# Four of the ten local row minima subtracted by GpSimd with one exponential for them, small copies moved to ScalarE, and the side work of VectorE placed behind the totals

## The chip, the core and the metric

The kernel runs on one NeuronCore of one Trainium2 chip. Five engines work side by side, each through its own instructions in program order: TensorE (PE, with its weight loads as PEld), VectorE (DVE), ScalarE (ACT), GpSimd (POOL), and SyncE (SP), which here only issues DMAs. They wait for each other through semaphores written out by hand. The metric is the time of the whole program in microseconds (us) on the device; lower is better. The kernel before took 819.59 us (median of three runs, 819.48 to 819.81).

## The reference

Three parts follow each other, all in float32. First comes attention over 4 batches x 8 heads, 576 positions, head size 64, in two forms that are added:

```python
q_d, k_d, v_d = (mean over groups of 4 positions of q, k, v)
out_d = sm_attn(q_d, k_d, v_d)              # 144 x 144 scores per head
out_up = np.repeat(out_d, factor, axis=2)
mask = np.abs(pos[:, None] - pos[None, :]) < factor      # a band of 7 keys
scores = np.where(mask, scale * q @ k^T, -1e9)
attn = exp(scores - max); attn /= (sum + 1e-9)
x = out_up + attn @ v
```

Then `h = (x @ w1) * (x @ w2) @ w3 @ w_out` on 2304 tokens of width 512 with inner width 1024, and last `silu(h @ w_in) @ w_out2` with inner width 2048.

## The kernel before, in words

**Layout.** Two heads are one pair, and there are 16 pairs. The attention is a software pipeline of 17 steps: in `step(s)` each engine does its share of pair s and the rest of pair s-1. Behind it run 48 sets of seven products (line 993) and the layers that follow them, which fill TensorE from about 165 us on. The product of `moe_w3` with `moe_w_out` is folded into the attention steps (line 1076), a twelve-matmul portion in each from step 4 on, so that TensorE has work there.

**The local attention of a pair** is computed on ten blocks of 64 queries by 64 keys (five groups of two per head; the tile `prob`, 128 x 640). DVE copies the negated, scaled scores out of PSUM and adds the mask (`mask_local`, line 718), and then takes the minimum of each block's rows (line 723, tile `low`, 128 x 10). ACT turns each of the ten blocks into exponentials with `low` as its bias and lets the accumulator add up the row (line 484, tile `tot`). DVE adds 1e-9 and inverts (`totals_local`, lines 739 and 741), POOL multiplies the whole tile by the inverse (line 402), PE transposes it (line 1128), ACT copies it back (`copy_pt`), and PE multiplies with the values (line 1151).

**The downsampled attention** goes the same way on a smaller scale: `qkd` from DVE (line 707), scores on PE (line 1095), maximum and its scaling on DVE (lines 729 and 733), four exponentials on ACT (line 473), totals on DVE (lines 746 and 749), the normalisation on POOL (line 408), transposes on PE (line 1120), `copy_ptd` on ACT, the product on PE (line 1137), a copy to `od` on DVE (`take_down`, line 753), and the sum of both forms into `x` (`take_local`, line 762).

**The order within one step** is fixed by the code:

- PE: local scores of pair s, downsampled scores of s, local transposes of s-1, nine fold matmuls, downsampled transposes of s-1, three fold matmuls, both products of s-1.
- DVE: x of pair s-2, mask and minimum of s, downsampled totals of s-1 (it makes `invd`), maximum of s, `qkd` of s+1, in some steps the two copies of a fold result (`take_w3o`) and one half of the first product's operands (table `EXTRA`), local totals of s, `od` of s-1.
- ACT: the fold's weights (`w3_high`), `copy_pt`, six local exponentials, `copy_ptd`, four local exponentials, four downsampled ones, in two steps a copy of weights for the first product (table `HIGHS`).
- POOL: sums over the values (lines 380 to 389), in eight steps a weight sum (line 364, table `SUMS`), the local normalisation of s, `w3_low` (line 369), the downsampled normalisation of s (line 408), which waits for `invd` from the next DVE step.

## Time and profile before

| what | us |
|---|---|
| median of the runs | 819.59 |
| the profiled execution | 821.13 |
| its span in the trace | 819.2 |
| PE busy (share) | 794.3 (97%) |
| DVE busy | 600.9 (73%) |
| ACT busy | 354.9 (43%) |
| POOL busy | 279.3 (34%) |

The profiled execution lies 1.54 us above the median of the runs, and 1.93 us of it lie outside the span. The page shows the span in 40 slices of 20.5 us. In the first seven, which hold the attention, DVE, ACT and POOL stand at 5 to 9 tenths and the DMA share at 3 to 8; after them PE stands at 9 and the rest falls off. TensorE's granted clock is at 9 tenths or more in every slice but the second (7 tenths).

```text
PE   7699899999999999999999999999999999999998
DVE  5898997687676776876669677679767769756644
ACT  6878877333352232443246323334422344432331
POOL 6778877432313333133213123113113212311100
PEclk9799999999999999999999999999999999999999
```

### The profile page before, as it was taken

The page shows a single profiled execution, that of the slowest core. Times are in us where ns is not written, and L with a number is a line of the kernel's source. Part 1 is how long each engine was busy: PE and PEld are TensorE (multiplying, and loading weights), DVE is VectorE, ACT ScalarE, POOL GpSimd, SP SyncE. Part 2 cuts the span into 40 slices and gives each one's busy share as a digit, 9 for nine tenths or more (in the row PEclk, how much of TensorE's full clock was granted, in tenths as well). Part 3 has the DMA queues.
Part 4 walks back from the last instruction along what each step waited for, and adds up shares of the span by engine and source line. Part 5 has one row for each costly group of instructions (what it writes and reads, how often), then busy time and mean ns, then how long its engine had stood idle before and what let it go on. Part 6 is the DMA issues. An engine that isn't in the chain of part 4 may idle for free.

```text
span 819.2 us, 13951 instructions
## 1 busy us (share of the span) xinstructions
PE 794.3 (97%) x5393; PEld 714.9 (87%) x5393; DVE 600.9 (73%) x957; ACT 354.9 (43%) x863; POOL 279.3 (34%) x342
## 2 busy tenths in 40 slices
PE   7699899999999999999999999999999999999998
PEld 6577777899999899999999889888888988988887
DVE  5898997687676776876669677679767769756644
ACT  6878877333352232443246323334422344432331
POOL 6778877432313333133213123113113212311100
PEclk9799999999999999999999999999999999999999
DMA  8475753011111111101103122122312112412102
GB/s 302 150 243 171 237 159 120 29 52 33 46 52 52 30 49 52 45 33 52 51 27 130 51 81 74 52 78 78 129 56 99 52 51 78 154 52 78 51 1 78
DMA packets 23041, 69.84 MB, mean 85 GB/s; under 512 B 2496, under 2 KB 2496, under 8 KB 22976
## 3 DMA queue, kind: packets, MB, share of 16 engines
q1 hardware_dynamic: 22832, 68.36, 25.7%
q8 instruction: 43, 0.70, 0.4%
q10 hardware_dynamic: 144, 0.59, 0.2%
q14 instruction: 22, 0.18, 0.1%
HBM read 64.23 MB, written 4.72 MB: 84 GB/s over the span
## 4 chain that ended last, share of the span: by engine, by line
PE 84%; POOL 5%; DVE 4%; DMA 2%; issue 2%; ACT 2%; SPq 0%; POOLq 0%
PE ps L993 42%; PE ps L1051 24%; PE ps L1022 12%; PE ps L1076 2%; DMA wn<-in_w 2%; POOL prob L402 2%; POOL w3t L369 1%; POOL prob_d L408 1%; PE ps L1120 1%; DVE wa L681 1%; PE ps L1151 1%; ACT prob L484 1%; POOL vd L385 1%; DMA qk<-in_qk 1%; PE ps L1137 1%
## 5 line engine op out<-in xcount | busy, mean ns | idle before, releaser
L993 PE MATMUL ps<-xb,wa 128*128 128x384 f32 x2016 | 406.9, 339 | 1.9 <-DVE a L821 1.4
L993 PEld LDWEIGHTS ps<-xb,wa 128*128 128x128 f32 x2016 | 356.6, 189 | 24.3 <-DVE a L821 2.1
L364 POOL TENSOR_TENSOR rw<-rw 128x256 f32<-128x256 f32 x192 | 167.9, 893 | 450.0 <-DMA rw<-in_sets 339.8
L821 DVE TENSOR_TENSOR mu<-ps,mu 128x384 f32<-128x384 f32 x132 | 73.2, 555 | 121.7 <-PE ps L993 121.2
L1022 PE MATMUL ps<-g,r 128*128 128x512 f32 (+1 forms) x576 | 124.9, 338 | 1.6 <-issue 1.6
L575 ACT ACTIVATE a<-a 128x384 f32<-128x384 f32 x72 | 37.9, 526 | 189.1 <-DVE a L821 189.1
L1051 PE MATMUL ps<-w2h_even,g 128*128 128x512 f32 x432 | 113.2, 394 | 0.0
L1051 PE MATMUL ps<-w2h_odd,g 128*128 128x512 f32 x432 | 112.5, 393 | 0.0
L681 DVE TENSOR_TENSOR wa<-rw,wa 128x1024 fp32r<-128x1024 f32 x96 | 107.0, 1114 | 3.0 <-ACT wa L427 2.7
L1022 PEld LDWEIGHTS ps<-g,r 128*128 128x128 f32 x576 | 97.7, 188 | 10.1 <-issue 2.2
L1051 PEld LDWEIGHTS ps<-w2h_odd,g 128*128 128x128 f32 x432 | 79.9, 188 | 11.9
L1051 PEld LDWEIGHTS ps<-w2h_even,g 128*128 128x128 f32 x432 | 79.9, 188 | 11.7
L821 DVE TENSOR_TENSOR a<-ps,mu 128x384 f32<-128x384 f32 x108 | 59.9, 555 | 37.2 <-PE ps L993 36.2
L427 ACT ACTIVATE wa<-rw 128x1792 fp32r<-128x1792 f32 (+2 forms) x49 | 81.5, 1663 | 0.0
L427 ACT ACTIVATE mu<-ps 128x384 f32<-128x384 f32 x48 | 23.3, 486 | 111.0 <-PE ps L993 111.0
L848 DVE TENSOR_TENSOR g<-a,g 128x384 fp32r<-128x384 f32 x96 | 64.1, 668 | 3.3
L427 ACT ACTIVATE g<-a 128x384 fp32r<-128x384 f32 x48 | 25.3, 526 | 80.2 <-DVE a L827 63.4
L484 ACT ACTIVATE prob<-prob,low 128x64 f32<-128x64 f32 x160 | 53.3, 338 | 6.9 <-DVE low L723 6.6
L1076 PE MATMUL ps<-r,w3t 128*128 128x512 f32 x192 | 51.0, 404 | 0.0
L846 DVE CAST g<-a 128x384 fp32r<-128x384 f32 x96 | 45.3, 472 | 0.0
L1076 PEld LDWEIGHTS ps<-r,w3t 128*128 128x128 f32 x192 | 34.0, 189 | 5.8
L833 DVE TENSOR_TENSOR g<-a,g 128x384 fp32r<-128x384 f32 x48 | 32.9, 690 | 0.4
(75 smaller groups left out, 744.2 us busy)
## 6 DMA issues: line engine op xcount, KB each, us to landing
rw<-in_sets SPq DMA_DIRECT2D x48, 512.0 KB, 3.6
w2r<-in_w_out SPq DMA_DIRECT2D x24, 512.0 KB, 3.5
qk<-in_qk SPq DMA_DIRECT2D x15, 576.0 KB, 5.5
vg<-in_vg SPq DMA_DIRECT2D x16, 336.0 KB, 6.0
vw<-in_vw SPq DMA_DIRECT2D x16, 320.0 KB, 3.0
out<-osb SPq DMA_DIRECT2D x18, 256.0 KB, 2.3
wn<-in_w SPq DMA_DIRECT2D x16, 256.0 KB, 5.1
raw<-in_w_out SPq DMA_DIRECT2D x2, 1024.0 KB, 9.5
```

Of the source, the lines that this page charges most:

```text
L364: nc.gpsimd.tensor_tensor(blocks[:, o, :], blocks[:, a, :], blocks[:, b, :], op).then_inc(done, 1)
L427: return nc.scalar.activation(o, a, ACT.Copy)
L484: e = nc.scalar.activation(pr, pr, ACT.Exp, bias=low[:, u, n:n + 1], scale=-1.0, accum_out=tot[:, u, n:n + 1])
L575: nc.scalar.activation(q, q, ACT.Silu).then_inc(g_act, 1)
L681: e = nc.vector.tensor_tensor(wa[:, k % 2, 1, blocks, :], rw[:, k % 2, 1 + blocks.start:1 + blocks.stop, :], wa[:, k % 2, 0, blocks, :].bi ...
L821: nc.vector.tensor_tensor(o, half_bank(k, i), term, ALU.add).then_inc(sum_ready, 1)
L846: nc.vector.tensor_copy(g[:, 0, j % 2, q // 2, to], a4[:, q, :]).then_inc(g_hi, 1)
L848: nc.vector.tensor_tensor(g[:, 1, j % 2, q // 2, to], a4[:, q, :], g[:, 0, j % 2, q // 2, to].bitcast(F32), ALU.subtract).then_inc(g_lo, 1)
L993: e = nc.tensor.matmul(ps[:, (k + i) % 2, 0:TH], wa[:, k % 2, l, A_SLOT[i], a * P:(a + 1) * P], xb[:, i, r, a, :], start=(i in (0, 1, 4) a ...
L1022: e = nc.tensor.matmul(o, r2[:, m + MT // 2 * f, l, b * P:(b + 1) * P], g[:, r, n % 2, f, to], start=(first and p == 0 and not (rest and b ...
L1051: e = nc.tensor.matmul(ps[:, 2 + tb, :], g[:, l, j % 2, q // 2, at], w2h[j % 2][:, q // 2, r, :], start=(c == 0 and a < 2 and p == 0), sto ...
L1076: e = nc.tensor.matmul(ps[:, fold_bank(q), :], w3t[:, l, a, :], r3[:, a, r, :], start=(a == 0 and p == 0), stop=(a == MT - 1 and p == 2))
```

## The change

Nothing changes on PE; the work moves among DVE, ACT and POOL inside the attention steps.

- **Local exponentials.** ACT now does only the first six blocks (groups 0 to 2) with bias and accumulator. For the last four (128 x 256) POOL subtracts `low` (`shift_local`), ACT takes one exponential over all of them, and DVE sums their rows (a TENSOR_REDUCE into `tot`). In POOL's order the subtraction for pair s+1 stands between `w3_low` and the downsampled normalisation of pair s.
- **Small copies.** The scaling of the downsampled maximum, the copy to `od` and the first copy of each fold result go from DVE to ACT, behind the late exponential.
- **Side work behind the totals.** On DVE the rest of `take_w3o` and the `EXTRA` halves come after `totals_local` instead of before it. The weight loads, weight sums and copies for the first product come one step earlier (`SUMS`, `HIGHS`), and `EXTRA` has a new order.

The core of the diff:

```diff
-        SUMS = (6, 10)
-        HIGHS = (8, 10)
-        EXTRA = {9: ("tokens", 0), 10: ("tokens", 1), 11: ("weights", 0), 12: ("tokens", 2), 13: ("weights", 1),
+        SUMS = (5, 9)
+        HIGHS = (7, 9)
+        EXTRA = {8: ("weights", 0), 10: ("tokens", 0), 11: ("weights", 1), 12: ("tokens", 1), 13: ("tokens", 2),
                  14: ("tokens", 3)}
...
+            def shift_local(s):
+                u = s % 2
+                pool.wait_ge(low_l, s + 1)
+                late = prob[:, u, LATE:NG, :, :].rearrange("p g h k -> p (g h) k")
+                nc.gpsimd.tensor_tensor(late, late, low[:, u, 2 * LATE:10, None].broadcast_to([P, 10 - 2 * LATE, BW]),
+                                        ALU.subtract).then_inc(shifted, 1)
...
+                if s == 0:
+                    shift_local(0)
+                    shift_local(1)
...
                 for q in splits_of(s + 1)[:1]:
                     w3_low(q)
+                if s > 0 and s + 1 < PAIRS:
+                    shift_local(s + 1)
                 pool.wait_ge(inv_d, s + 1)
...
                 def exps_down():
+                    act.wait_ge(maxd, s + 1)
+                    nc.scalar.activation(lowd16[:, u, :], lowd[:, u, :], ACT.Copy, scale=-D ** -0.5 / POOL ** 2
+                                         ).then_inc(low_d, 1)
                     act.wait_ge(low_d, s + 1)
...
+                def exps_late():
+                    act.wait_ge(shifted, s + 1)
+                    late = prob[:, u, LATE:NG, :, :].rearrange("p g h k -> p (g h k)")
+                    nc.scalar.activation(late, late, ACT.Exp, scale=-1.0).then_inc(exp_s, 1)
+
+                def take_down():
+                    act.wait_ge(summed_d, s)
+                    after(act, x_ready, 2 * (s - 2))
+                    copy_act(od[:, (s - 1) % 2, :], ps[:, pO, 0:SD]).then_inc(od_ready, 1)
...
+                if s > 2:
+                    exps_local()
+                if s > 0:
+                    copy_ptd()
+                if s == 2:
+                    exps_local()
+                if s != 1:
+                    exps_late()
+                for q in halves_of(s):
+                    if q % 2 == 1:
+                        take_w3o(q // 2)
...
                 exps_down()
+                if s > 0:
+                    take_down()
...
             def totals_local(s):
                 u = s % 2
+                dve.wait_ge(exp_s, s + 1)
+                nc.vector.tensor_reduce(tot[:, u, 2 * LATE:10].rearrange("p (g h) -> p g h", h=2),
+                                        prob[:, u, LATE:NG, :, :], AX.X, ALU.add).then_inc(sum_l, 1)
                 dve.wait_ge(exp_l, s + 1)
+                dve.wait_ge(sum_l, s + 1)
...
+                totals_local(s)
+                if s == 0:
+                    totals_down(0)
                 for q in halves_of(s):
                     if q % 2 == 1:
                         take_w3o(q // 2)
...
-                totals_local(s)
-                if s == 0:
-                    totals_down(0)
-                else:
-                    take_down(s - 1)
```

On POOL, in the steps with a weight sum, these rows stood before (`w3t` is `w3_low`, the second `prob` row's place is the local normalisation, `prob_d` the downsampled one, `vt` the next pair's values):

```order
L364 TENSOR_TENSOR rw<-rw 128x256
L402 TENSOR_TENSOR prob<-prob,inv 128x640
L369 TENSOR_TENSOR w3t<-wn,w3t 128x512
L408 TENSOR_TENSOR prob_d<-prob_d,invd 72x4x144
L380 TENSOR_TENSOR vt<-vg 112x384
```

And these stand there now:

```order
L367 TENSOR_TENSOR rw<-rw 128x256
L415 TENSOR_TENSOR prob<-prob,inv 128x640
L372 TENSOR_TENSOR w3t<-wn,w3t 128x512
L380 TENSOR_TENSOR prob<-prob,low 128x256
L423 TENSOR_TENSOR prob_d<-prob_d,invd 72x4x144
L390 TENSOR_TENSOR vt<-vg 112x384
```

One row is new, the subtraction, directly ahead of the downsampled normalisation. On ACT, a step with a fold result read before (`pt` and `ptd` are the copies of the transposes, the last row opens the next step):

```order
L427 ACTIVATE pt<-ps 128x384
L427 ACTIVATE pt<-ps 128x256
L484 ACTIVATE prob,tot<-prob,low 128x64 x6
L427 ACTIVATE ptd<-ps 112x2x3x72
L484 ACTIVATE prob,tot<-prob,low 128x64 x4
L473 ACTIVATE prob_d,totd<-ps,lowd 72x144 x4
L427 ACTIVATE w3t<-wn 128x512
```

The same step now, here one that also holds the weight copy of `HIGHS` (step 7):

```order
L442 ACTIVATE pt<-ps 128x384
L442 ACTIVATE pt<-ps 128x256
L506 ACTIVATE prob,tot<-prob,low 128x64 x6
L442 ACTIVATE ptd<-ps 112x2x3x72
L513 ACTIVATE prob<-prob 128x256
L442 ACTIVATE r<-ps 128x512
L490 ACTIVATE lowd<-lowd 72x4
L495 ACTIVATE prob_d,totd<-ps,lowd 72x144 x4
L442 ACTIVATE od<-ps 128x144
L442 ACTIVATE wa<-rw 128x1024
L442 ACTIVATE w3t<-wn 128x512
```

Four blocks became one row, and three small rows came in around the downsampled exponentials. On DVE, a step with a fold result and an `EXTRA` half, from `qkd` to the next `x`, read before (step 11):

```order
L707 TENSOR_REDUCE qkd<-qk 128x288
L698 CAST r<-ps 128x512
L700 TENSOR_TENSOR r<-ps,r 128x512
L681 TENSOR_TENSOR wa<-rw,wa 128x1024
L739 TENSOR_SCALAR tot<-tot 128x10
L741 RECIPROCAL inv<-tot 128x10
L753 COPY od<-ps 128x144
L762 TENSOR_TENSOR x<-ps,od 128x288 x2
```

And now:

```order
L743 TENSOR_REDUCE qkd<-qk 128x288
L772 TENSOR_REDUCE tot<-prob 128x4
L776 TENSOR_SCALAR tot<-tot 128x10
L778 RECIPROCAL inv<-tot 128x10
L736 TENSOR_TENSOR r<-ps,r 128x512
L719 TENSOR_TENSOR wa<-rw,wa 128x768
L795 TENSOR_TENSOR x<-ps,od 128x288 x2
```

The totals moved ahead of the side work, which now stands directly in front of the next step's `x`; two copies left.

## Rows read from the trace of the kernel before

**Rows 1.** Windows: us, busy us per engine (instructions), PEclk, DMA share, GB/s.

```profile
45.00:60.00 15.00, 14.11 (x230) 11.64 (x228) 14.18 (x29) 12.34 (x60) 12.19 (x17) 1.00 0.66 213
180.00:195.00 15.00, 15.00 (x86) 14.23 (x85) 9.37 (x15) 3.13 (x4) 3.36 (x5) 1.00 0.23 71
```

**Rows 2.** Waits, 45 to 135 us: us in total, times, longest.

```profile
PEld ps L1120 <- POOL prob_d L408: 6.0, 11, 1.1
```

**Rows 3.** Timeline, step 6: start us, us, engine, line, operation, out<-in.

```profile
56.13 0.27 PE L1108 MATMUL ps<-qk 64*64 64x64 f32 x1
56.53 0.82 DVE L762 TENSOR_TENSOR x<-ps,od 128x288 f32<-128x288 f32 x2 [0.36 <-PE ps L1151]
58.18 0.82 DVE L723 TENSOR_REDUCE low<-prob 128x10 f32<-128x640 f32 x1
58.21 1.30 POOL L369 TENSOR_TENSOR w3t<-wn,w3t 128x512 fp32r<-128x512 f32 x1 [0.80 <-ACT w3t L427]
58.92 0.62 DVE L746 TENSOR_SCALAR totd<-totd 72x4 f32<-72x4 f32 x1
59.82 1.14 POOL L408 TENSOR_TENSOR prob_d<-prob_d,invd 72x576 f32<-72x576 f32 x1 [0.31 <-DVE invd L749]
62.07 0.34 ACT L484 ACTIVATE prob<-prob,low 128x64 f32<-128x64 f32 x1
63.40 0.36 ACT L473 ACTIVATE prob_d<-ps,lowd 72x144 f32<-72x144 f32 x1
63.53 0.58 DVE L739 TENSOR_SCALAR tot<-tot 128x10 f32<-128x10 f32 x1 [1.28 <-ACT prob L484]
64.26 0.27 PE L1108 MATMUL ps<-qk 64*64 64x64 f32 x1
64.82 0.63 ACT L427 ACTIVATE w3t<-wn 128x512 fp32r<-128x512 f32 x1
```

**Rows 4.** Timeline, starts in steps 5, 7, 8 and 15.

```profile
47.78 0.27 PE L1108 MATMUL ps<-qk 64*64 64x64 f32 x1
48.88 1.26 POOL L402 TENSOR_TENSOR prob<-prob,inv 128x640 f32<-128x640 f32 x1
...
67.05 0.16 DVE L746 TENSOR_SCALAR totd<-totd 72x4 f32<-72x4 f32 x1
67.49 1.14 POOL L408 TENSOR_TENSOR prob_d<-prob_d,invd 72x576 f32<-72x576 f32 x1 [0.56 <-DVE invd L749]
71.93 0.27 PE L1108 MATMUL ps<-qk 64*64 64x64 f32 x1
...
129.53 0.27 PE L1108 MATMUL ps<-qk 64*64 64x64 f32 x1
132.76 1.14 POOL L408 TENSOR_TENSOR prob_d<-prob_d,invd 72x576 f32<-72x576 f32 x1 [0.67 <-DVE invd L749]
```

**Rows 5.** Groups by shape, 45 to 135 us: busy us, mean ns, idle before.

```profile
L402 POOL TENSOR_TENSOR prob<-prob,inv 128x640 f32<-128x640 f32 x11 | 13.9, 1259 | 6.2 <-DVE inv L741 6.0
L364 POOL TENSOR_TENSOR rw<-rw 128x256 f32<-128x256 f32 x8 | 5.8, 729 | 0.6
L427 ACT ACTIVATE pt<-ps 128x256 f32<-128x256 f32 x11 | 4.2, 379 | 0.0
```

**Rows 6.** Timeline around 94 us.

```profile
94.11 1.84 POOL L385 TENSOR_TENSOR vd<-vt 96x64 f32<-96x64 f32 x3
94.27 0.94 DVE L675 TENSOR_TENSOR tr<-x,tr 128x768 f32<-128x768 f32 x1
```

**Rows 7.** Timeline, steps 2 and 3.

```profile
29.07 0.82 DVE L762 TENSOR_TENSOR x<-ps,od 128x288 f32<-128x288 f32 x2
29.31 0.38 ACT L473 ACTIVATE prob_d<-ps,lowd 72x144 f32<-72x144 f32 x1
33.16 1.14 POOL L408 TENSOR_TENSOR prob_d<-prob_d,invd 72x576 f32<-72x576 f32 x1
```

**Rows 8.** Windows of the start.

```profile
33.00:45.00 12.00, 10.03 (x121) 8.70 (x121) 9.55 (x16) 8.84 (x43) 9.65 (x12) 0.65 0.34 114
```

More of the change, by code:

```diff
@@ L170, in attention_then_mlps @@
             sem("pooled"), sem("maxd"), sem("low_d"), sem("masked"), sem("low_l"), sem("x_ready"))
+        shifted, exp_s, sum_l = sem("shifted"), sem("exp_s"), sem("sum_l")
         added_d, added_l, inv_d, inv_l = sem("added_d"), sem("added_l"), sem("inv_d"), sem("inv_l")
@@ L180, in attention_then_mlps @@
         s1_ready, s2_ready, s3_ready, s4_ready = sem("s1_ready"), sem("s2_ready"), sem("s3_ready"), sem("s4_ready")
-        wa_hi, wa_lo = sem("wa_hi"), sem("wa_lo")
+        wa_hi, wa_lo, wa_first = sem("wa_hi"), sem("wa_lo"), sem("wa_first")
         prod, m1_ready, sum_ready, c11_taken = sem("prod"), sem("m1_ready"), sem("sum_ready"), sem("c11_taken")
@@ L452, in first_weights_high @@
                     act.wait_ge(s1_ready, 1)
-                    copy_act(wa[:, 0, 0, 0:4, :], rw[:, 0, 1:5, :])
+                    copy_act(wa[:, 0, 0, 0:4, :], rw[:, 0, 1:5, :]).then_inc(wa_first, 1)
                 else:
@@ L457, in first_weights_high, with take_w3o @@
                     copy_act(wa[:, 0, 0, 4:7, :], rw[:, 0, 5:8, :]).then_inc(wa_hi, 1)
+            def take_w3o(m):
+                act.wait_ge(w3_mul, 2 * m + 2)
+                copy_act(r2[:, m, 0, :], ps[:, fold_bank(2 * m), :]).then_inc(w3o_hi, 1)
             def w3_high(q):
@@ L477, in exps_down, with exps_local @@
                     e.then_inc(exp_d, 1)
-                def exps_local(groups):
+                def exps_local():
                     act.wait_ge(low_l, s + 1)
-                    for g in groups:
+                    for g in range(LATE):
                         for h in range(2):
@@ L514, in step @@
                     tokens_high(0, 2)
+                    take_w3o(MT - 2)
                     w3_high(HALVES - 1)
+                    take_down()
                     act.wait_ge(w3_lo, HALVES)
@@ L522, in step @@
                     tokens_high(0, 6)
+                    take_w3o(MT - 1)
                     return
@@ L526, in step @@
                     w3_high(q)
+                if s < 2:
+                    exps_local()
+                if s == 1:
+                    exps_late()
+                if s > 0:
+                    copy_pt()
+                if s > 2:
[3 more added lines that the diff above has]
+                if s == 2:
+                    exps_local()
+                if s != 1:
+                    exps_late()
+                for q in halves_of(s):
+                    if q % 2 == 1:
+                        take_w3o(q // 2)
                 if s == 0:
-                    exps_local(range(NG))
                     act.wait_ge(blank, 2)
-                elif s == 1:
-                    exps_local(range(LATE))
-                    copy_pt()
-                    copy_ptd()
-                    exps_local(range(LATE, NG))
-                elif s == 2:
-                    copy_pt()
-                    copy_ptd()
-                    exps_local(range(NG))
-                else:
-                    copy_pt()
-                    exps_local(range(LATE))
-                    copy_ptd()
-                    exps_local(range(LATE, NG))
                 exps_down()
+                if s > 0:
+                    take_down()
                 for n in W_OUT.get(s, ()):
@@ L678, in weights_low @@
                 blocks = (slice(0, 4), slice(4, 7))[half]
-                if half == 0:
+                if half == 0 and k > 0:
                     dve.wait_ge(wa_hi, k + 1)
@@ L731, in max_down @@
                                         AX.X, ALU.max).then_inc(maxd, 1)
-                dve.wait_ge(maxd, s + 1)
-                nc.vector.tensor_scalar(lowd16[:, u, :], lowd[:, u, :],
-                                        -D ** -0.5 / POOL ** 2, None, ALU.mult).then_inc(low_d, 1)
             def totals_local(s):
                 u = s % 2
+                dve.wait_ge(exp_s, s + 1)
+                nc.vector.tensor_reduce(tot[:, u, 2 * LATE:10].rearrange("p (g h) -> p g h", h=2),
+                                        prob[:, u, LATE:NG, :, :], AX.X, ALU.add).then_inc(sum_l, 1)
                 dve.wait_ge(exp_l, s + 1)
+                dve.wait_ge(sum_l, s + 1)
                 nc.vector.tensor_scalar(tot1[:, u, :], tot[:, u, :], 1e-9, None, ALU.add).then_inc(added_l, 1)
@@ L793, in step @@
                     else:
+                        if n == 0:
+                            dve.wait_ge(wa_first, 1)
+                        else:
+                            dve.wait_ge(wa_hi, 1)
                         weights_low(0, n)
-                totals_local(s)
-                if s == 0:
-                    totals_down(0)
-                else:
-                    take_down(s - 1)
             pool_pair(0)
@@ L809, in _ @@
             take_w3o(MT - 2)
-            take_down(PAIRS - 1)
             take_local(PAIRS - 1)
```

8 lines of the change are left out of this document (1 added, 7 removed).

## The prediction

> **What bounds the kernel now.** I read the windows first. From 180 us on TensorE is busy 15.00 of 15.00 us, while in the attention it is busy 14.11 of 15 [rows 1]. The change touches only the attention and its two ends, so what is to win or lose lies there. The waits tell what TensorE lacks: its loads of the downsampled transposes wait for POOL's downsampled normalisation in all of eleven steps [rows 2]. The timeline tells how this sets the pace.
>
> I call S the start of a step's local scores on PE and N the start of the downsampled normalisation (L408) inside that step. In step 6, S is 56.13, N is 59.82 and the next S is 64.26 [rows 3]: N comes 3.69 us after S, and the next S 4.44 us after N. In step 7, S is 64.26, N 67.49 and the next S 71.93 [rows 3, 4]: 3.23 and again 4.44. In each of the ten steps from 5 to 14 it is 4.44 within 0.01, whatever DVE and ACT had beside it. So a step lasts L + 4.44, with L the lag from S to N, and the attention is priced by L alone. Ten steps take 129.53 - 47.78 = 81.75 us [rows 4], so their ten lags sum to 81.75 - 44.4 = 37.35; step 15 adds 132.76 - 129.53 = 3.23. The eleven lags sum to 40.6, 3.69 each, with 3.23 the shortest.
>
> What makes up L is seen in step 6 [rows 3]: `x` of pair s-2 starts 0.40 us after S (the end of the previous products), the row minimum starts at 2.05 and ends at 2.87, then come the downsampled totals on DVE, `invd`, and N. In step 7 the totals take 0.16 us and N is 0.36 after the minimum's end [rows 4]; in step 6 they take 0.62 [rows 3], because `w3_low` runs on POOL until 59.51 and the totals end only at 59.54.
>
> **The late exponentials.** Four blocks take 63.40 - 62.07 = 1.33 us on ACT [rows 3]. One instruction of 256 elements took 0.38 as a copy [rows 5]; I take 0.42 for the exponential. DVE's new sum over 256 elements is 256/640 of the minimum's 0.82, 0.33, to 0.43 with a fixed part; I take 0.43. Local totals come 0.5 us earlier. This is worth nothing by itself: the local normalisation feeds the local transposes and `w3_low`, and neither of them is what PE waits for last. In step 6 everything local is over before the wait at N.
>
> **The subtraction on POOL.** 256 elements cost between 0.50 (256/640 of 1.26) and 0.73 (the 128x256 weight sum) [rows 5]; I take 0.60. It cannot start before the minimum of pair s+1 is done, and it stands in front of N. So a step that is otherwise on time has N at 2.87 + 0.05 + 0.60 + 0.03 = 3.55 after S, where the best one now has 3.23. What hid behind it before, totals and `invd`, took 0.36. Both ends: 3.45 to 3.68. Nothing covers it, since PE already waits at exactly this place.
>
> **The small copies on ACT.** Counted from N: `copy_ptd` is over at 62.07 - 59.82 = 2.25 [rows 3]. Then come the late exponential (0.42), in odd steps the first fold copy (512 elements, 0.60 from the 0.38 of 256 [rows 5]), the scaled maximum with its hand-over (0.30, by the smallest ACT rows 0.2 each), four downsampled exponentials (64.82 - 63.40 = 1.42 [rows 3]), and the copy to `od` (0.28). It ends at N + 4.67 in even steps and N + 5.27 in odd ones. The next `x` starts at N + 4.44 + 0.40 = 4.84 today and needs `od`. So behind even steps nothing is late; behind odd steps it starts at about 5.35, 0.5 late, and with it mask, minimum, subtraction and N. Lags of steps 6, 10, 12, 14 and 8 become 4.05. In steps 8 and 10 the weight copy of `HIGHS` (1024 and 768 elements, by the 0.63 of 512 [rows 3] some 1.06 and 0.85 us) stands between the copy to `od` and `w3_high`, so `w3_low` and with it the subtraction come later still: ACT is through `w3_high` at N + 5.27 + 1.06 + 0.63 = 6.96, `w3_low` ends at 8.3, which is 3.9 after S, and N is at 4.55 (step 8), by the same count 4.35 (step 10). In step 12 DVE itself, behind a fold result and a weight half, is through only about 0.1 after ACT; I leave it at 4.05. Even steps: 3 x 4.05 + 4.55 + 4.35 = 21.05.
>
> **The side work behind the totals.** DVE's row of totals, counted from N: the late exponential is over at 2.67, the sum at 3.15, and `inv` is ready at 3.6, if the small totals instruction is not held up. In step 6 it was: it took 0.58 us instead of 0.16 [rows 3], beside a weight sum on POOL. If it is held until the weight sum ends, `inv` is ready at N + 4.55. Then the `EXTRA` half (0.94 for tokens [rows 6], up to 1.3 for 1024 elements of weights) is behind it and ends at 5.0 to 6.0, past the 4.84 at which the next `x` is due. In the kernel before this time lay where DVE waited for the exponentials anyway, in the even steps. Steps 9, 11 and 13 have such a half in front: unhindered totals give 3.75, 3.55, 3.55, held-up totals 4.65, 4.3, 4.15. A token half beside a POOL instruction also stretched three short additions to 1.84 us [rows 6], which speaks for the later ones. I take values about halfway: 4.1, 3.9, 3.85. Step 5 is bound by POOL: the local normalisation starts 1.10 after S [rows 4], it and `w3_low` (1.26 and 1.30) end 3.6 after S, and the subtraction follows: 4.3. Steps 7 and 15 have 3.55. Odd steps: 4.3 + 3.55 + 4.1 + 3.9 + 3.85 + 3.55 = 23.25.
>
> The Trainium skill, page "SBUF — State Buffer", section "Who interferes with whom", says that VectorE's tensor_scalar in a two-port mode and a GpSimd instruction lock each other out of a shared pair of ports for a whole instruction, and that an addition with both inputs in SBUF contends with GpSimd's reads. The rows of the totals (0.16 alone, 0.58 and 0.62 beside POOL) and the 1.84 us [rows 3, 4, 6] agree. By that rule the subtraction, which follows `w3_low` without a gap, could also keep the downsampled totals out until it has ended, which is the third rival's price.
>
> **The start.** In steps 2 and 3 ACT is the engine that is never idle. The downsampled exponentials of step 2 end about 29.67, the copy to `od` now comes after them, and `x` starts at about 29.85 instead of 29.07 [rows 7]: 0.78 late. The subtraction's excess over the totals' 0.36 adds 0.3 and the one in step 2 shifts the row before by another 0.3. N of step 3, now 33.16 [rows 7], comes 1.1 to 1.4 later; I take 1.4. In the window from 33 to 45 us the granted clock reads 0.65 [rows 8]: some 8.4 of the 12 us at its lower level, 1.2 GHz, beginning while PE waits for this N. I expect the same stretch again.
>
> **The end.** After the last step ACT reaches `w3_high` 0.35 later than now, behind the same fold copy and `od`; the rest of the way to the first products is PE's and DVE's own and unchanged: 0.35.
>
> **The sum.** Steps 5 to 15: 21.05 + 23.25 - 40.6 = +3.7. Start +1.4, end +0.35. Together +5.45 on the profiled 821.13, so 826.6; the profile lies 1.54 above the median, and against 819.59 this is 825.0.
>
> **The rivals.**
>
> *Faster: the gain of even distribution.* The mean lag stands 0.46 over the shortest, since in some steps DVE comes late from side work and in others the totals wait for `w3_low`, as in step 6. If ACT keeps up (its copies cost less than I count) and the totals are never held up, every lag is 3.45: 11 x 3.45 = 37.95, which is 2.65 less than 40.6. If besides PE is kept busy enough at the start for the clock not to fall, the twelve us of [rows 8] lose about 2 us of slow matmuls. That gives 815 to 817. For it: DVE loses the scaling, a copy and half of a fold result, against a sum of 0.43. Against it: in no step does the subtraction vanish, and `x` behind odd steps needs ACT to save 0.5 us. 15 in 100 including its milder forms.
>
> *No change.* The late steps recover (-1.5 to -2.6) and the start pays 1.0 to 1.4: 818.5 to 820. It needs the same on ACT as the first rival. 15 in 100.
>
> *Slower still: the totals are starved.* If the downsampled totals are held out behind `w3_low` and the subtraction in every step where `w3_low` runs until the minimum's end, they and `invd` add 0.3 us after the subtraction in six or seven steps (+2), and the held-up values of steps 9, 11 and 13 add 1.25: 828.3. It decides from the point where `w3_low` ends later than 2.87 after S. 20 in 100.
>
> *That the change doesn't do what it says* would show in POOL's order, and the rows of the order have the subtraction where the code puts it.
>
> **How the numbers follow.** The forecast, 822 to 827 around 825.0, has 50 in 100. Faster than before by over 0.2% (1.6 us, about what can be told from no change here) is 0.15, within it 0.15, slower 0.70. The range goes from 817.5, which takes in no change and the mild half of the first rival, to 829, which takes in the starved case. The forecast's own range is 822 to 827.
>
> **What the changed profile would show.** Right: N minus S at 3.5 or more in every step from 5 to 15, next S still N + 4.44; `x` waiting for ACT's `od` in steps 6, 8, 10, 12 and 14; POOL's subtraction at about 0.6 us directly ahead of N. Wrong: lags under 3.4 (the subtraction is cheaper or hidden), a distance from N to the next S that differs from 4.44 (something else than N sets the pace), or no half clock near 35 us.

## The result and the profile after

The changed kernel takes 822.75 us (median of seven runs, 822.29 to 824.02); the kernel before took 819.81 in the seven runs beside it (819.46 to 822.24). The ratio is 1.0032, with a 95% interval from 1.0020 to 1.0044: slower by 2.6 to 2.9 us. The forecast was 825.0 and "slower"; the direction held, the size is about half of the 5.45 us that was summed up. The profiled execution is itself one of 822.75 us, with a span of 821.0 (before: 819.2).

The page shows that work has moved as the diff says: POOL gained 9.8 us of busy time, DVE lost 9.6 and ACT 5.8.

```profile
span 821.0 us, 13901 instructions
PE 792.2 (97%) x5393; PEld 712.1 (87%) x5393; DVE 591.3 (72%) x933; ACT 349.1 (43%) x791; POOL 289.1 (35%) x358
```

The windows of the changed kernel that answer to [rows 1, 8] (columns as there). From 180 us on nothing changed. In the attention PE is busy 0.43 us less of the 15, and POOL 1.59 more. Half clock at the start came again, shorter (0.72 against 0.65).

```profile
33.00:45.00 12.00, 9.11 (x114) 7.64 (x114) 10.06 (x18) 8.12 (x37) 10.11 (x13) 0.72 0.36 118
45.00:60.00 15.00, 13.68 (x229) 11.21 (x230) 12.00 (x23) 11.14 (x48) 13.78 (x19) 1.00 0.62 199
180.00:195.00 15.00, 15.00 (x86) 14.18 (x85) 9.31 (x14) 3.13 (x4) 2.88 (x4) 1.00 0.24 71
```

The wait of [rows 2], 45 to 135 us, in the changed kernel. TensorE's loads still wait eleven times for POOL's downsampled normalisation, now 9.3 us in place of 6.0:

```profile
PEld ps L1154 <- POOL prob_d L423: 9.3, 11, 1.2
```

Step 6 in the changed kernel's timeline, against [rows 3] (start, us, engine, line, operation):

```profile
57.08 0.27 PE L1142 MATMUL ps<-qk 64*64 64x64 f32 x1
57.37 0.28 ACT L442 ACTIVATE od<-ps 128x144 f32<-128x144 f32 x1
57.68 0.82 DVE L795 TENSOR_TENSOR x<-ps,od 128x288 f32<-128x288 f32 x2 [0.76 <-ACT od L442]
...
60.07 0.16 DVE L783 TENSOR_SCALAR totd<-totd 72x4 f32<-72x4 f32 x1
60.24 0.62 POOL L380 TENSOR_TENSOR prob<-prob,low 128x256 f32<-128x256 f32 x1 [0.71 <-DVE low L759]
60.81 1.15 POOL L423 TENSOR_TENSOR prob_d<-prob_d,invd 72x576 f32<-72x576 f32 x1
...
65.25 0.27 PE L1142 MATMUL ps<-qk 64*64 64x64 f32 x1
...
68.04 0.16 DVE L783 TENSOR_SCALAR totd<-totd 72x4 f32<-72x4 f32 x1
...
68.77 1.15 POOL L423 TENSOR_TENSOR prob_d<-prob_d,invd 72x576 f32<-72x576 f32 x1
```

S is 57.08, `x` waits for ACT's `od` and starts 0.60 after S (before 0.40), the subtraction runs 0.62 directly ahead of N, N is 60.81, and the next S, 65.25, is N + 4.44. Step 7 is the best one: N at 68.77 is 3.52 after S, where it was 3.23 [rows 3, 4]. The totals take 0.16 in both: they get in before the subtraction.

The groups by shape of the changed kernel, 45 to 135 us, beside [rows 5] (busy us, mean ns of one, idle before):

```profile
L415 POOL TENSOR_TENSOR prob<-prob,inv 128x640 f32<-128x640 f32 x11 | 17.6, 1601 | 0.9 <-DVE inv L778 0.9
L380 POOL TENSOR_TENSOR prob<-prob,low 128x256 f32<-128x256 f32 x11 | 6.8, 616 | 3.6 <-DVE low L759 3.2
L772 DVE TENSOR_REDUCE tot<-prob 128x4 f32<-128x256 f32 x11 | 4.6, 419 | 11.4 <-ACT prob L513 11.4
L513 ACT ACTIVATE prob<-prob 128x256 f32<-128x256 f32 x11 | 4.5, 408 | 0.0
L442 ACT ACTIVATE od<-ps 128x144 f32<-128x144 f32 x11 | 3.1, 285 | 0.0
L442 ACT ACTIVATE r<-ps 128x512 fp32r<-128x512 f32 x5 | 3.0, 597 | 0.0
L783 DVE TENSOR_SCALAR totd<-totd 72x4 f32<-72x4 f32 x11 | 2.6, 240 | 0.0
L490 ACT ACTIVATE lowd<-lowd 72x4 f32<-72x4 f32 x11 | 2.1, 193 | 0.0
```

Every new operation has the price that was forecast (0.62 for 0.60, 0.41 for 0.42, 0.42 for 0.43, 0.29 for 0.28, 0.60 for 0.60). What has grown is the local normalisation, 1259 to 1601 ns in the mean.

**The balance by steps.** The lag is S to N, read from the timeline (last digits rounded):

| step | 5 | 6 | 7 | 8 | 9 | 10 | 11 | 12 | 13 | 14 | 15 | sum |
|---|---|---|---|---|---|---|---|---|---|---|---|---|
| before | 3.91 | 3.69 | 3.23 | 3.30 | 3.82 | 4.00 | 3.60 | 4.26 | 3.57 | 4.01 | 3.23 | 40.6 |
| forecast | 4.3 | 4.05 | 3.55 | 4.55 | 4.1 | 4.35 | 3.9 | 4.05 | 3.85 | 4.05 | 3.55 | 44.3 |
| changed | 4.02 | 3.73 | 3.52 | 3.95 | 3.94 | 3.73 | 3.68 | 3.74 | 3.68 | 4.57 | 3.52 | 42.1 |
| `x` after S | .40 | .60 | .40 | .61 | .83 | .60 | .57 | .62 | .57 | 1.45 | .39 | |

From N to the next S it is 4.43 or 4.44 in each step from 5 to 14. Against the span's start, the two timelines differ so: the first S came 0.49 later (6.54 against 6.05; it waits for the DMA of `qk`, which the change does not touch, and lies between 5.86 and 6.61 in the fourteen profiles of this document), the way from there to step 5 grew by 0.36 (42.09 against 41.73), the lags by 1.46, and the way from N of step 15 (135.10 against 132.76) to the last downsampled normalisation by 0.26. That makes 2.6, of which 0.5 is not the change's. Then the trace of before loses some of it by itself: its granted clock falls once more at the first products. The two traces there, before first (windows as above):

```profile
160.00:162.00 2.00, 1.22 (x4) 1.22 (x5) 1.19 (x3) 0.00 (x0) 1.92 (x3) 0.74 0.31 72
162.00:164.00 2.00, 2.00 (x7) 2.00 (x7) 0.56 (x1) 0.00 (x0) 0.53 (x2) 0.50 0.48 190
```

```profile
160.00:162.00 2.00, 1.82 (x9) 1.18 (x8) 2.00 (x4) 0.00 (x0) 1.44 (x2) 1.00 0.00 0
162.00:164.00 2.00, 0.73 (x4) 0.73 (x5) 1.68 (x3) 0.00 (x0) 2.00 (x2) 1.00 0.21 25
```

The first sets' `a` start 2.5 us apart (160.2 and 162.7), those at 166.8 and 167.8 still 1.0. So 1.5 us of the difference is missing there, because the profiled execution of before had this second stretch; none of the thirteen other profiles has one at this place. That execution, 821.13, also lay 1.3 to 1.5 above the medians of its kernel. Of the 2.6 to 2.9 us between the medians the change's own rows explain 2.1 (0.36 + 1.46 + 0.26, without the later first S); the rest, 0.5 to 0.8, has no row. That is the grain of such a balance: from the first matmul of the sets to the last of `w2h_even`, work that no kernel here changes, the profiles take 653.2 to 654.2 us (654.8 in before's), and below, attention and median differ by up to 1.2 us either way.

### The profile page after: what moved, and what is told of

It is laid out like the page before. It is cut to its first block, busy times and chain, and to the rows that moved or that the text cites. A ratio compares the mean times of both kernels' runs of the same rounds, so it can differ in the third digit from the quotient of the medians.

```text
span 821.0 us, 13901 instructions
## 1 busy us (share of the span) xinstructions
PE 792.2 (97%) x5393; PEld 712.1 (87%) x5393; DVE 591.3 (72%) x933; ACT 349.1 (43%) x791; POOL 289.1 (35%) x358
## 4 chain that ended last, share of the span: by engine, by line
PE 83%; DVE 6%; ACT 4%; POOL 3%; issue 2%; DMA 2%; SPq 0%; DVEq 0%; POOLq 0%; ACTq 0%
PE ps L1027 42%; PE ps L1085 24%; PE ps L1056 12%; POOL prob_d L423 2%; PE ps L1110 1%; PE ps L1154 1%; DVE low L759 1%; DVE prob L754 1%; ACT prob_d L495 1%; DMA wn<-in_w 1%; PE ps L1185 1%; DVE x L795 1%; ACT ptd L442 1%; DVE wa L719 1%; DMA qk<-in_qk 1%
## 5 line engine op out<-in xcount | busy, mean ns | idle before, releaser
L506 ACT ACTIVATE prob<-prob,low 128x64 f32<-128x64 f32 x96 | 32.1, 338 | 8.3 <-DVE low L759 8.1
```

## The experiments

The twelve kernels were timed against the kernel before in four sets (e1 to e4, e5 to e8, e9 to e11, e12); the median of before was 820.81, 820.16, 820.23 and 820.32 in them, and 819.81 beside the changed kernel. So medians of different sets are up to 1.0 us apart for nothing, and the ratios are the safer comparison. "Start" is from the first S to S of step 5 (41.73 before, 42.09 changed), "lags" the sum of steps 5 to 15.

| kernel | median | ratio (95%) | start | lags | shortest lag |
|---|---|---|---|---|---|
| changed | 822.75 | 1.0032 (1.0020 to 1.0044) | 42.09 | 42.1 | 3.52 |
| e1 | 821.22 | 1.0003 (0.9994 to 1.0012) | 41.28 | 41.8 | 3.23 |
| e2 | 822.80 | 1.0029 (1.0017 to 1.0040) | 41.87 | 42.7 | 3.52 |
| e3 | 825.61 | 1.0059 (1.0046 to 1.0071) | 43.19 | 43.6 | 3.52 |
| e4 | 830.17 | 1.0116 (1.0103 to 1.0130) | 43.49 | 47.7 | 3.95 |
| e5 | 825.25 | 1.0062 (1.0049 to 1.0075) | 41.82 | 44.6 | 3.52 |
| e6 | 827.45 | 1.0084 (1.0071 to 1.0098) | 41.43 | 46.7 | 3.23 |
| e7 | 820.64 | 1.0006 (0.9997 to 1.0014) | 40.79 | 40.8 | 3.23 |
| e8 | 820.61 | 1.0001 (0.9992 to 1.0010) | 40.76 | 40.6 | 3.23 |
| e9 | 819.33 | 0.9989 (0.9980 to 0.9998) | 41.61 | 39.2 | 3.23 |
| e10 | 818.47 | 0.9977 (0.9968 to 0.9986) | 40.14 | 39.4 | 3.23 |
| e11 | 817.80 | 0.9971 (0.9960 to 0.9983) | 39.90 | 40.3 | 3.23 |
| e12 | 819.67 | 0.9995 (0.9986 to 1.0004) | 39.90 | 41.7 | 3.23 |

**e1_shift_behind: the subtraction behind the downsampled normalisation.** From the changed kernel, on POOL:

```diff
                 for q in splits_of(s + 1)[:1]:
                     w3_low(q)
-                if s > 0 and s + 1 < PAIRS:
-                    shift_local(s + 1)
                 pool.wait_ge(inv_d, s + 1)
...
                                         ).then_inc(norm_d, 1)
+                if s > 0 and s + 1 < PAIRS:
+                    shift_local(s + 1)
```

> The changed kernel with one edit: POOL's subtraction for pair s+1 stands behind the downsampled normalisation of pair s instead of in front of it. In the changed kernel the start of that normalisation (N) comes 3.52 us or more after the start of the local scores (S), where the kernel before had 3.23. Theory 1 (the subtraction in front of N is what lengthens the steps): the shortest lag goes back to 3.23, the eleven lags of steps 5 to 15 lose about 0.25 us each, and with the start the kernel gains about 3 us: 819.5 to 820. Theory 2 (the copies on ACT and the side work on DVE are what counts): the lags stay where they are and the time stays at 822.5. Against theory 1 speaks only that the values and the local normalisation on POOL come 0.6 us later, which nobody waits for last.

It took 821.22, by its ratio level with the kernel before (1.0003), as expected. The shortest lag is back at 3.23, so the subtraction is what lifted it by 0.29 (0.32 was forecast). But the trace shows less than the "0.25 us in each of eleven lags": the start is 0.8 shorter and the lags as a whole fell by 0.3 only, 1.1 us together where the ratios are 2.4 us apart. In steps 5, 9 and 11 to 13 the lags rose. Step 11 of this kernel, with S at 96.74:

```profile
97.77 1.25 POOL L415 TENSOR_TENSOR prob<-prob,inv 128x640 f32<-128x640 f32 x1
98.98 1.27 POOL L372 TENSOR_TENSOR w3t<-wn,w3t 128x512 fp32r<-128x512 f32 x1
99.53 0.75 DVE L783 TENSOR_SCALAR totd<-totd 72x4 f32<-72x4 f32 x1
100.57 1.14 POOL L421 TENSOR_TENSOR prob_d<-prob_d,invd 72x576 f32<-72x576 f32 x1 [0.32 <-DVE invd L786]
```

The local normalisation starts 1.03 after S (the subtraction delays the exponential, that delays `inv`, and a weight sum comes in between), `w3_low` runs until 100.25, and the downsampled totals take 0.75 instead of 0.16. The gain of 0.29 per step turned into a wait for `w3_low`.

**e2_extra_front: the halves ahead of the local totals.** From the changed kernel, on DVE:

```diff
+                if s in EXTRA: ...          # the whole block
                 totals_local(s)
...
-                if s in EXTRA: ...
```

> The changed kernel with the halves for the first product (table EXTRA) ahead of the local totals on DVE again, the fold result's second half still behind them. Theory 2: step 14, whose lag is 4.57 us in the changed kernel with x 1.45 us after S, falls to about 3.6, step 9 from 3.94 to 3.7, and the local normalisation on POOL takes 1.26 us again in steps 8 and 10 to 12 where it now takes 2.0: 1.3 to 2 us gained, 821. Theory 1: these halves were only a small part, 0.5 us or less gained.

It took 822.80, no different from the changed kernel. Step 14 fell from 4.57 to 3.73, and POOL's local normalisation takes 1.26 us again in every step, both as expected. But `inv` came later, and with it POOL's local normalisation and `w3_low`. Step 11 of this kernel, with S at 98.17:

```profile
100.38 1.29 POOL L372 TENSOR_TENSOR w3t<-wn,w3t 128x512 fp32r<-128x512 f32 x1
100.95 0.74 DVE L783 TENSOR_SCALAR totd<-totd 72x4 f32<-72x4 f32 x1
...
102.20 1.15 POOL L423 TENSOR_TENSOR prob_d<-prob_d,invd 72x576 f32<-72x576 f32 x1
```

The totals (0.74) are kept out beside `w3_low`, the subtraction follows them, and the lag is 4.03, not 3.68. Steps 9 and 11 to 13 rose by 0.29 to 0.35 each. So both orders on DVE cost the same, in other steps, and the forecast's term "halves behind totals" bought nothing that could be had back by undoing it.

**e3_od_on_dve: the copy to `od` back on DVE, at the end of its row.**

```diff
-                if s > 0:
-                    take_down()                       # ACT
...
+                if s > 0:
+                    take_down(s - 1)                  # DVE, behind the EXTRA half
```

> The changed kernel with the copy to od back on DVE, at the end of its step. In the changed kernel x starts 0.60 us after S in steps 6, 8, 10 and 12 and 0.40 in steps 7 and 15, where only ACT's od is in the way. If ACT's lateness is the cause (theory 2, copies): these four go to 0.40 and the kernel gains 0.8 to 1 us: 822. If the copies cost what the prediction had (0.5 us in each of five steps): 2.5 us. Theory 1: under 0.5 us, since DVE's own row ends little earlier.

A gain of about 1 us was expected; it took 2.9 us more (2.2 by the ratios). Steps 6 and 10, the ones where only ACT's `od` was late, fell by 0.2 as expected (3.73 to 3.53 and 3.54). In steps 9 and 11 to 14 the copy stands behind the fold result and the half, and `x` starts 0.88 to 1.77 after S. The other part of the loss is at the start, which is 1.10 longer: N to the next S takes 7.89 us in step 3, where it was 6.49. At that place on DVE the copy costs more than ACT's late one; where it costs nothing is seen in e7.

**e4_no_subtraction: ten exponentials on ACT again, all else as changed.** This kernel keeps the small copies and the side order, without `shift_local`, the joint exponential and DVE's sum over it:

```diff
-                if s > 0 and s + 1 < PAIRS:
-                    shift_local(s + 1)
...
                 def exps_late():
-                    act.wait_ge(shifted, s + 1)
-                    late = prob[:, u, LATE:NG, :, :].rearrange("p g h k -> p (g h k)")
-                    nc.scalar.activation(late, late, ACT.Exp, scale=-1.0).then_inc(exp_s, 1)
+                    exps_local(range(LATE, NG))       # bias and accumulator, as before
```

> The changed kernel without the subtraction and the joint exponential: ACT does all ten local blocks with bias and accumulator as before, the sum on DVE is gone; copies on ACT and side work behind the totals stay. Theory 1 taken alone: the shortest lag returns to 3.23, 3 us gained. Both theories together: ACT then spends 1.33 us where it spends 0.41, the copy to od comes 0.9 us later (N + 5.6 in even and N + 6.2 us in odd steps against the 4.84 at which x is due), every lag becomes 4.0 to 4.6 although the subtraction is gone, and the kernel is slower than the changed one: 826 to 828.

It took 830.17, 9.4 above before. In step 6 of this kernel, with S at 58.71:

```profile
59.99 0.28 ACT L437 ACTIVATE od<-ps 128x144 f32<-128x144 f32 x1
60.31 0.82 DVE L785 TENSOR_TENSOR x<-ps,od 128x288 f32<-128x288 f32 x2 [0.94 <-ACT od L437]
```

ACT reaches `od` 1.28 after S, where it is 0.29 in the changed kernel: `x` starts 1.60 or more after S behind odd steps and 1.12 behind even ones, where it was mostly 0.60 and 0.40. In step 1 PE also waits 1.50 us for ACT's `ptd`, and the next S comes 5.94 after N. The 0.9 us that the joint exponential saves on ACT (1.33 to 0.41) is what makes room for the copies.

**e5_late_only: the kernel before with the subtraction, the joint exponential and the sum alone.**

```diff
+                if s > 0 and s + 1 < PAIRS:
+                    shift_local(s + 1)                # before's POOL, ahead of the wait for invd
...
+                        nc.scalar.activation(late, late, ACT.Exp, scale=-1.0).then_inc(exp_s, 1)
```

> The kernel before with the joint exponential alone: the subtraction on POOL in front of the downsampled normalisation, one exponential for four blocks, the sum on DVE; all small copies stay on DVE, side work and tables as before. Theory (the subtraction sets the floor, DVE's row sets the rest): shortest lag from S to N 3.52 instead of 3.23; in steps 10, 12 and 14 the new sum of 0.42 us stands behind the side work and in front of x, so that their lags grow by about 0.7. In all +3.5 to +4.5 against the kernel before, more than the whole change costs (+2.6): 824. Rival (the joint exponential is a gain that the other parts spoil): at or under the kernel before.

825.25, 5.1 above before. The shortest lag is 3.52 again. Steps 10, 12 and 14 rise to 4.83, 5.10 and 4.83: DVE, with the sum added to its row, starts `x` 1.70 to 1.97 after S.

**e6_side_only: the kernel before with the side order and its tables alone.**

```diff
+                totals_local(s)
+                if s == 0:
+                    totals_down(0)
+                else:
+                    take_down(s - 1)
                 for q in halves_of(s):
...
-                totals_local(s)                       # and take_down, from the end of the row
```

> The kernel before with the third part alone: fold results and EXTRA halves behind the local totals and the copy to od on DVE, tables as in the changed kernel; ten exponentials on ACT, both fold copies on DVE. Theory: without the copies that went to ACT, DVE has 1.3 us of fold copies and 1 us of halves behind the totals, x starts about 1.4 us after S instead of 0.4 in steps 6, 8 and 10 and later in 12 and 14: +4 to +6, 825. Rival (earlier totals are a gain for the local chain): no slower than before.

827.45, 7.3 above before, more than expected. With ten exponentials on ACT the totals come late and the side work later still. Step 12 of this kernel has its S at 107.39:

```profile
108.89 1.97 DVE L681 TENSOR_TENSOR wa<-rw,wa 128x768 fp32r<-128x768 f32 x1
110.79 0.81 DVE L762 TENSOR_TENSOR x<-ps,od 128x288 f32<-128x288 f32 x2
```

The weight half takes 1.97 beside POOL, and `x` starts 3.40 after S; the lag is 6.22. PE sits idle for 2.83 us there until `x` has started, the granted clock then falls (0.54 from 112 to 114 us, 0.61 from 114 to 116), and the next S comes 5.57 after N.

e4 to e6 show that the parts do not add: +5.1 for one, +7.3 for another, +9.4 for all but the first, and +2.9 together. The joint exponential pays for the copies on ACT, and these free DVE for the sum and for side work behind the totals. The copies alone, on the kernel before, were not run.

**e7_behind_od_dve and e8_behind_od_extra.** e7 is e1 with `od` on DVE right behind the local totals; e8 is e7 with the halves ahead of the totals.

```diff
                 totals_local(s)
+                if s > 0:
+                    take_down(s - 1)                  # DVE; e8: and the EXTRA block ahead of totals_local
```

> The changed kernel with the subtraction behind the downsampled normalisation and the copy to od on DVE right behind the local totals, ahead of the fold result and the halves. The first gives the shortest lag 3.23 as it did alone; the second takes x back to 0.40 in steps 6, 8 and 10 (-0.2 each) and adds 0.25 in front of the halves. Sum of the eleven lags about 41.5: 820.5 to 821, unless the start loses 1.4 us as it did with od at the end of DVE's row, where 7.9 us passed from N to the next S in step 3 instead of 6.5.

> The same as the run beside it, with the halves for the first product ahead of the totals too. Step 14, whose lag was 4.48 with the halves behind, falls to about 3.5; steps 9, 11 and 13 stay at 3.8 to 4.1, because the local normalisation starts 1.0 us after S there and the downsampled totals are held out while w3_low runs. Sum of the lags about 40.7, level with the kernel before: 820 to 820.5.

820.64 and 820.61, both level with before. With the subtraction out of POOL's way and `od` in time, steps 6, 7 and 8 are at 3.23, 3.23 and 3.55; steps 9 and 11 to 13 stay at 3.75 to 4.3 in both. In e8 the reason is plain: `w3_low` there ends 3.7 to 4.0 after S and the totals take 0.91 to 1.21 us, against 0.16 to 0.28 in steps 7 and 14. Both attentions are about 0.9 us shorter at the start and at most 0.3 longer later, yet the medians only equal before's. The profiled executions took 819.70 and 819.64, 0.9 and 1.0 under the medians of their kernels, so the traces show fast ones; where the others lose this 1 us no run tells.

**e9_weight_sums_late: e8 with POOL's weight sums behind `w3_low`.**

```diff
-                for k in range(2): ... weight_sum(k, s - SUMS[k])     # ahead of the local normalisation
...
                     w3_low(q)
+                for k in range(2): ... weight_sum(k, s - SUMS[k])
                 pool.wait_ge(inv_d, s + 1)
```

> The last version (subtraction behind the downsampled normalisation, od on DVE behind the totals, halves ahead of them) with POOL's weight sums moved from in front of the local normalisation to behind w3_low. In steps 9, 11, 12 and 13 N comes 4.0 to 4.3 us after S because the local totals wait for the weight sum to end, the local normalisation starts at 1.2, w3_low runs until 3.7 and keeps the downsampled totals out. Theory (POOL's row, not DVE's, delays these steps): the local normalisation starts at about -0.1, w3_low ends by 2.5, the weight sum fills POOL's wait up to 3.2, and the four lags fall to 3.3 to 3.5: 2.5 us less than the last version, 818. Rival (the halves on DVE delay them): the lags stay over 3.9.

819.33: 1.3 better than e8 (1.0 by the ratios), half of what was expected or less. Step 11 of this kernel, S at 96.03:

```profile
97.63 1.28 POOL L372 TENSOR_TENSOR w3t<-wn,w3t 128x512 fp32r<-128x512 f32 x1
98.86 0.16 DVE L780 TENSOR_SCALAR totd<-totd 72x4 f32<-72x4 f32 x1
98.87 0.74 POOL L367 TENSOR_TENSOR rw<-rw 128x256 f32<-128x256 f32 x1
99.57 1.15 POOL L421 TENSOR_TENSOR prob_d<-prob_d,invd 72x576 f32<-72x576 f32 x1
```

`w3_low` is now through when the totals are due, and these take 0.16. But the weight sum stands where the subtraction stood, directly ahead of N, and N is 3.54 after S, not 3.23. Steps 8 and 10 rose by about 0.35 for the same reason.

**e10_late_warm and e11_before_warm: idle transposes in step 3.** `warm(n)` issues n transposes whose result nobody reads; steps 1 and 2 of before already have them. e10 adds the edit to e9, e11 adds it to the kernel before and nothing else.

```diff
-                warm({1: 30, 2: 6}.get(s, 0))
+                warm({1: 30, 2: 6, 3: 10}.get(s, 0))
...
-                    warm({1: 4, 2: 6}.get(s, 0))
+                    warm({1: 4, 2: 6, 3: 20}.get(s, 0))
...
-                    warm({1: 5, 2: 6}.get(s, 0))
+                    warm({1: 5, 2: 6, 3: 5}.get(s, 0))
```

> The run beside it with idle transposes on PE in step 3 as there are in steps 1 and 2 (10, 20 and 5 of them), which write only a bank of PSUM that nothing uses yet. In step 3 PE waits some 1.5 us for the downsampled exponentials and 3 us for N, the granted clock falls to 0.50 there in every version, and 6.4 us pass from N to the next S instead of 4.44. Theory: with PE busy the clock stays at 1.00 and the step gives back 1.9 us: 816. Rival: the clock falls anyway or the transposes themselves come late, no gain or a loss of up to 1 us.

> The kernel before with the same idle transposes in step 3 and nothing else. Theory: N to the next S falls from 6.49 to 4.44 us in step 3: 818. Rival: as beside it.

818.47 and 817.80. The window from 30 to 42 us of before and of e11, in this order:

```profile
30.00:42.00 12.00, 8.36 (x114) 7.12 (x115) 9.55 (x17) 9.33 (x38) 9.31 (x11) 0.57 0.33 103
```

```profile
30.00:42.00 12.00, 10.19 (x150) 8.80 (x150) 11.76 (x21) 10.73 (x45) 9.80 (x12) 1.00 0.49 156
```

The granted clock stays at its upper level. In e11's timeline N of step 3 is at 33.12, where it was 33.16 [rows 7], and the next S follows after 4.44 us, not 6.49:

```profile
33.12 1.15 POOL L408 TENSOR_TENSOR prob_d<-prob_d,invd 72x576 f32<-72x576 f32 x1
37.56 0.27 PE L1108 MATMUL ps<-qk 64*64 64x64 f32 x1
```

Before, the half clock cost 2.05 us in step 3 alone; of these step 4 gives 0.24 back as a longer lag (3.68 to 3.92). The start is 39.90 against 41.73. e11 is the fastest kernel here, 0.29% under before and, by the two ratios, 0.6% under the changed kernel. In e10 the start won 1.5 against e9, not the full 2.05, because the lag of step 4 rose from 3.68 to 4.55 (there POOL's own row comes next) and only 0.29 of that came back behind N. The median won 0.9; of the other 0.6 the later lags hold 0.2, the rest has no row.

**e12_before_warm_sums: e11 with e9's weight sums behind `w3_low`.** The edit is the one of e9, on the kernel before.

> The kernel before with the idle transposes in step 3 and, beside them, POOL's weight sums behind w3_low. With the transposes alone the eleven lags are 40.27: steps 11 and 13 stand at 3.57 to 3.60 because w3_low keeps the downsampled totals out (they take 0.50 to 0.53 us instead of 0.16), steps 10, 12 and 14 at 4.0 to 4.3 because DVE's own row brings x late. Theory: the first two fall to about 3.35, the last three stay; 0.5 us less than with the transposes alone, 817.3. Rival (weight sums in front of N delay it wherever DVE is on time, since nothing but POOL's wait hides them): steps 7 and 8 rise from 3.23 to 3.5 or more and the kernel is no faster, 818.

819.67, 1.9 slower than e11, which was timed in another set (ratios 0.9995 and 0.9971, 2.0 us apart). Its lags sum to 41.7 against 40.3. Step 8 of this kernel, S at 70.12:

```profile
72.62 0.74 POOL L364 TENSOR_TENSOR rw<-rw 128x256 f32<-128x256 f32 x1
72.91 0.48 DVE L746 TENSOR_SCALAR totd<-totd 72x4 f32<-72x4 f32 x1
73.67 1.14 POOL L408 TENSOR_TENSOR prob_d<-prob_d,invd 72x576 f32<-72x576 f32 x1 [0.31 <-DVE invd L749]
```

The totals take 0.48 beside the weight sum, N waits for the `invd` behind them and is 3.55 after S instead of 3.23. The same 0.3 us as for the subtraction, from another instruction at the same place, here by way of the totals.

## Why the prediction was right, and where its size failed

**Lag plus 4.44: right.** From step 5 on the next S comes 4.43 to 4.45 after N in all fourteen profiles, with one exception: 5.57 in step 12 of e6, at a fallen clock. Before step 5 it is more in step 3 (6.23 to 7.89, at the start's half clock; 4.44 where the idle transposes kept the clock up), in step 4 of e9 (4.73) and in step 1 of e4 (5.94). That let every kernel here be read from one list of lags and its start.

**The subtraction ahead of N: right, and shown.** Forecast 3.55 for the best step, measured 3.52. e1 takes it away and gets 3.23; e5 adds it alone and gets 3.52.

**Prices of single operations: right,** within 0.02 us for five of the six; the scaled maximum was 0.19, forecast at 0.30 with its hand-over.

**`od` 0.5 us late behind odd steps: mis-sized.** It is 0.2. In step 5 N is 52.65, and `od` ends at N + 5.00, not at N + 5.27; `x` starts at 0.60 after S, not at 0.9. The forecast added up each row of ACT from N with 0.30 for the scaled maximum and its hand-over. In the timeline ACT's rows overlap by about 0.1: the fold copy runs from 55.21 for 0.60, the scaled maximum from 55.70 for 0.19, so it moves the end of ACT's row by 0.08. Steps 6, 10 and 12 came out at 3.73 or 3.74 where 4.05 and 4.35 stood. The late `w3_high` of steps 8 and 10 was over-counted in the same way: ahead of step 8 it ends at N + 6.49, not N + 6.96, and `w3_low` ends 3.4 after S, not 3.9. Together these four steps hold 1.85 us of the 2.2 by which the lags missed.

**Held-up totals in steps 9, 11 and 13: did not happen.** From step 6 on the local normalisation starts 0.21 to 0.55 us before S in every step, so `inv` was ready by N + 4.2 at the latest (its own row ends at N + 3.75, S - 0.69), where held-up totals would have given N + 4.55. Of the values put halfway between unhindered and held up, the unhindered ones (3.75, 3.55, 3.55) are nearer to 3.94, 3.68 and 3.68. The third rival, totals starved by `w3_low` and the subtraction, shows only in steps 5 and 8 (0.72 and 0.45 us); the mean of eleven is 0.24, and was 0.37 before.

**Step 14: under-forecast, 4.57 against 4.05.** The trace of the changed kernel at the end of step 13:

```profile
122.03 1.26 POOL L415 TENSOR_TENSOR prob<-prob,inv 128x640 f32<-128x640 f32 x1 [0.42 <-DVE inv L778]
122.34 1.76 DVE L713 TENSOR_TENSOR tr<-x 128x768 f32<-128x768 f32 x1
122.57 0.27 PE L1142 MATMUL ps<-qk 64*64 64x64 f32 x1
124.02 0.81 DVE L795 TENSOR_TENSOR x<-ps,od 128x288 f32<-128x288 f32 x2
```

The token half behind the totals took 1.76 us beside POOL's normalisation and `w3_low`, where the forecast had 0.94 [rows 6]. It had charged halves to steps 9, 11 and 13, weighed one in step 12 and left out that of step 14, although `EXTRA` has one in step 13. So `x` of step 14 did not wait for ACT's `od`, as the forecast's signs had it, but for DVE's own row. e2 puts the half in front and gets 3.73 here.

**The start: 0.36 instead of 1.4.** The step before rose by 0.30 as forecast (lag 3.53 for 3.23). In step 3 `x` was only 0.14 later (2.09 after S against 1.95), not 0.78, and N did not move at all (6.01 for 6.04): it had stood behind `w3_low`, which ended 6.08 after S and now ends at 5.47, since ACT, with fewer exponentials, brings its half 0.6 earlier. The subtraction and totals of 1.02 us fill just that gap. `w3_low` of step 3 before, then the rows of the changed kernel (S 27.93, N 33.94):

```profile
31.94 1.26 POOL L369 TENSOR_TENSOR w3t<-wn,w3t 128x512 fp32r<-128x512 f32 x1 [1.66 <-ACT w3t L427]
```

```profile
32.14 1.26 POOL L372 TENSOR_TENSOR w3t<-wn,w3t 128x512 fp32r<-128x512 f32 x1 [1.50 <-ACT w3t L442]
32.41 1.02 DVE L783 TENSOR_SCALAR totd<-totd 72x4 f32<-72x4 f32 x1
33.37 0.61 POOL L380 TENSOR_TENSOR prob<-prob,low 128x256 f32<-128x256 f32 x1
```

The forecast had added the delays of this step and none of its savings. The end was 0.26 for 0.35.

**The offset of 1.54: right to subtract.** The second stretch of half clock at 161 to 165 us, which the other profiles lack, is worth about as much (1.5). The granted clocks of all executions speak for it too: of before's 76 in the four sets, the eight with a mean of 0.992 or less, the value of the profiled one, took 821.8 us on average, the other 68 took 820.3. That it is the cause is likely, not shown.

**What of the hit is luck.** The rows of the change explain 2.1 us, which from a median of 819.6 or 819.8 makes 821.7 to 821.9, just under the forecast's 822 to 827. The measured 822.75 lies inside by the 0.5 to 0.8 us that have no row. And the terms erred both ways: step 14 was 0.5 too low, while steps 6, 8, 10 and 12 were 1.85 and the start 1.0 too high.

So the step that failed is the arithmetic on ACT's and DVE's slack: delays were added link by link, while the savings of the same change on the same engines (1.33 to 0.41 on ACT, the copies gone from DVE) were followed only as far as the next row, not to `w3_high` and `w3_low` of the start or to `inv`. e4 and e5 show how large these savings are: 6.9 and 2.5 us by the ratios between each partial kernel and the whole (1.0116 and 1.0062 against 1.0032).

## What to carry to other kernels

When a software pipeline starts each step at a fixed distance behind one instruction, list that instruction's lag in every step and price a change by it: an instruction put directly ahead of it on its engine costs what of its time nothing else hides (0.3 us per step here, whether it was the subtraction or a weight sum), however idle that engine is on the page. Judge parts of a change that feed each other together, with savings and delays on the same engine's row in one sum. And look at the granted clock of the start first: 35 idle transposes in one step were worth more than all the reordering tried here.

## What the runs showed of the hardware

- **Two-input VectorE work and GpSimd stretch each other.** The token half takes 0.94 us in [rows 6], where POOL's three short additions are the ones stretched (1.84 us; 0.87 or 0.88 in steps 5 to 9 of before, which have no half beside them), and 1.76 in step 14. The weight half of 128x768 takes 0.94 in e2 and 1.97 in e6's step 12. POOL's local normalisation took 1.80 to 2.24 in place of 1.26 in five steps of the changed kernel, and 1.26 in every step of e2, where the halves stand elsewhere. Here step 11 of the changed kernel:

```profile
97.37 1.43 DVE L713 TENSOR_TENSOR tr<-x 128x768 f32<-128x768 f32 x1
97.94 1.98 POOL L415 TENSOR_TENSOR prob<-prob,inv 128x640 f32<-128x640 f32 x1
```

- **A very small instruction can wait over a whole large one.** The downsampled totals (72x4) take 0.16 us alone, 0.75 in e1's step 11, and 1.02 in the changed kernel's step 3. Each time they end 0.02 to 0.03 us after `w3_low`, which runs beside them.

- **The clock.** With idle transposes in PE's waits of step 3 the granted clock stayed at 1.00 where it had been 0.57 over twelve us. At the first products, from 161 us on, it fell to 0.50 in one profile of fourteen, that of before, although PE of the changed kernel is idle there as long (busy 2.55 of the 4 us from 160 on; before, the same work, 2.54 of the 4 us from 158 on). In e6 it fell at another place, in step 12, behind a wait of PE of 2.83 us. What decides it was not settled; no run was made for it.
